# Routing work of VectorE in two parts around the normalisation, and an earlier load of the third expert's weights, in an attention, mixture-of-experts and MLP kernel

## The reference

```python
# attention: 4 batches, 8 heads, 576 positions, head size 64, causal window of 64
scores = (1/8) * q @ k^T, masked to 0 <= i - j < 64
x = softmax(scores) @ v                      # gathered to 2304 tokens x 512
# mixture of experts, 8 experts, 512 -> 1024 -> 512
do_compute = x @ w_skip > 0
e_idx = argmax(x[do_compute] @ w_gate)       # first of equal ones
gate_w = softmax(logits)[e_idx]
y = gate_w * relu(x @ w1[e]) @ w2[e]         # for the tokens of expert e
x = x + y on the tokens with do_compute, x elsewhere
# MLP, 512 -> 2048 -> 512
h = x @ w_in;  out = (h * clip(h + 3, 0, 6) / 6) @ w_out
```

## Time and profile before

| | |
|---|---|
| median of three runs | 718.98 us (718.35 to 719.72) |
| the profiled execution's own time | 716.1 us |
| its span | 714.5 us |
| mean granted TensorE clock | 0.985 |
| TensorE matmul busy | 660.7 us, 92% |
| VectorE busy | 253.6 us, 35% |
| ScalarE busy | 241.3 us, 34% |

### The profile page before, as it was taken

The page is one execution under the profiler, slowest core; times in us unless marked ns, Lnnn a source line. Parts: engine busy times, 40 slices in busy tenths (PEclk is TensorE's granted clock), DMA queues, the critical chain, the costliest instruction groups (busy, mean ns, idle before and its releaser), DMA issues.

```text
span 714.5 us, 17144 instructions
## 1 busy us (share of the span) xinstructions
PE 660.7 (92%) x6662; PEld 580.1 (81%) x6662; DVE 253.6 (35%) x810; ACT 241.3 (34%) x571; POOL 71.6 (10%) x121
## 2 busy tenths in 40 slices
PE   5887776687999999999999999999999999999998
PEld 4776665575788787799989999999999899989996
DVE  2677665400111111265543224322422242224222
ACT  3786766111111111265433223222322232223221
POOL 5224343311111111100000000000000000000000
PEclk9999999898999999999999999999999999999999
DMA  6887768829948335445411002000200020001001
GB/s 151 182 198 176 195 173 281 312 69 380 362 152 304 123 122 201 134 119 147 146 53 38 0 1 89 0 0 0 88 0 0 0 89 0 0 0 44 1 1 44
DMA packets 97251, 78.13 MB, mean 109 GB/s; under 512 B 61793, under 2 KB 76901, under 8 KB 97200
## 3 DMA queue, kind: packets, MB, share of 16 engines
q1 hardware_dynamic: 83392, 43.20, 22.2%
q10 hardware_dynamic: 11360, 30.02, 11.8%
q0 software_dynamic: 2448, 4.22, 1.7%
HBM read 63.23 MB, written 17.52 MB: 113 GB/s over the span
## 4 chain that ended last, share of the span: by engine, by line
PE 79%; DMA 6%; DVE 4%; SPq 4%; issue 3%; ACT 2%; ACTq 1%; POOLq 0%; POOL 0%; DVEq 0%
PE bank L761 28%; PE bank L774 19%; PE av L774 9%; PE av L735 7%; PE bank L724 7%; DMA xin<-x_rows 3%; SPq L364 2%; PE av L621 2%; DMA kraw<-in_k 1%; PE bank L635 1%; ACT pr L820 1%; DVE xall L990 1%; PE bank L569 1%; SPq L372 1%; PE av L694 1%
## 5 line engine op out<-in xcount | busy, mean ns | idle before, releaser
L923 ACT ACTIVATE rel<-bank,half 128x384 f32<-128x384 f32 x96 | 55.7, 580 | 185.2 <-PE bank L761 185.2
L1112 DVE SCALAR_TENSOR_TENSOR act<-rel,bank 128x384 f32<-128x384 f32 x96 | 53.2, 554 | 169.9 <-ACT rel L923 169.9
L761 PE MATMUL bank<-xT_hi,wi_hi 128*128 128x384 f32 x384 | 83.3, 339 | 0.7 <-ACT xT_hi L916 0.7
L761 PE MATMUL bank<-xT_hi,wi_lo 128*128 128x384 f32 x384 | 82.9, 337 | 0.0
L761 PE MATMUL bank<-xT_lo,wi_hi 128*128 128x384 f32 x384 | 82.0, 334 | 0.0
L1116 DVE TENSOR_TENSOR g_lo<-act,g_hi 128x384 fp32r<-128x384 f32 x96 | 53.6, 558 | 67.2 <-ACT g_hi L934 67.2
L774 PE MATMUL bank<-wo_hi,g_lo 128*128 128x512 f32 x192 | 76.2, 397 | 0.0
L774 PE MATMUL bank<-wo_hi,g_hi 128*128 128x512 f32 x192 | 76.1, 396 | 0.0
L774 PE MATMUL bank<-wo_lo,g_hi 128*128 128x512 f32 x192 | 75.8, 395 | 0.0
L761 PEld LDWEIGHTS bank<-xT_hi,wi_hi 128*128 128x128 f32 x384 | 69.0, 188 | 7.7 <-ACT xT_hi L916 0.9
L934 ACT CAST g_hi<-act 128x384 fp32r<-128x384 f32 x96 | 49.3, 513 | 65.5 <-DVE act L1112 65.5
(11 more groups left out here) (123 smaller groups left out, 793.0 us busy)
## 6 DMA issues: line engine op xcount, KB each, us to landing
w1s<-in_moe_w ACTq DMA_DIRECT2D x7, 2048.0 KB, 9.0
w2s<-in_moe_w ACTq DMA_DIRECT2D x7, 2048.0 KB, 15.0
qraw<-in_q SPq DMA_DIRECT2D x36, 128.0 KB, 3.3
kraw<-in_k SPq DMA_DIRECT2D x36, 128.0 KB, 3.7
vnow<-in_v SPq DMA_DIRECT2D x36, 128.0 KB, 3.3
x_new<-xall SPq DMA_DIRECT2D x18, 256.0 KB
out<-ot SPq DMA_DIRECT2D x18, 256.0 KB, 2.1
xn<-x_new SPq DMA_DIRECT2D x17, 256.0 KB, 3.5
```

Of the source, the lines that this page charges most:

```text
L761: last = pe.matmul(bank[f % 4][:, 0:GN], a[:, f, c, :], b[:, c, :], start=(n == 0), stop=(n == 3 * DC - 1))
L923: sc.activation(rel[f % 2][:, :], bank[f % 4][:, 0:GN], ACT.Relu, scale=1.0 / 6.0, bias=half[:, :]).then_inc(s_rel, 1)
L1112: dve.scalar_tensor_tensor(out=act[f % 2][:, :], in0=rel[f % 2][:, :], scalar=1.0, in1=bank[f % 4][:, 0:GN], op0=ALU.min, op1=ALU.mult).th ...
```

## The change

- `choose` is cut in two: `choose` (the maximum, the differences `ldl`, the comparison `leq`) stays before `normalise`; the rest, now `assign` (L1009 to L1014 of before), comes after `normalise` in the same step.
- `place` is cut in two: `count` (for the last group the gate, then the ranks and the running total, L1033 and L1035) stays where `place` was; the rest, still `place` (L1036, L1037, the gate, L1041), comes after `normalise` in the same step.
- The transposed logits of the last three tiles go to banks 2 and 3 instead of bank 7, and no longer wait for `s_x`; `transpose_xs` of the last tile moves behind `logits` in its step.
- At the start, `transpose_qk(1)`, `take_q(1)` and `take_k(1)` move behind the scores, exponentials and score reduction of tile 0.
- ScalarE issues the two weight loads of expert 2 ahead of the loop over the experts, after a wait for `s_xin` to reach 64 (two tiles of `xin` have landed) in place of the wait for `s_scat`; two loads are left after expert 0.

```diff
@@ tensor
             def transpose_lg(T):
                 pe.wait_ge(s_lgs, T + 1)
-                pe.wait_ge(s_x, min(T + 3, NT))
-                if T >= NT - 2:
-                    pe.wait_ge(s_lgc, T)
-                pe.transpose(bank[7][:, LT:LT + P], lgs[:, :], ident[:, :]).then_inc(s_lgt, 1)
+                if T < NT - 3:
+                    pe.wait_ge(s_x, T + 3)
+                else:
+                    pe.wait_ge(s_sm, HP * NT)
+                    pe.wait_ge(s_lgc, T - 1)
+                pe.transpose(lg_bank(T)[:, LT:LT + P], lgs[:, :], ident[:, :]).then_inc(s_lgt, 1)
             transpose_qk(0)
-            transpose_qk(1)
             for T in range(NT + 5):
                 if T < NT:
                     scores(T)
+                if T == 0:
+                    transpose_qk(1)
...
-                if exists(T - 2, NT):
+                if exists(T - 2, NT - 1):
                     transpose_xs(T - 2)
                 if exists(T - 3, NT):
                     logits(T - 3)
+                if T - 2 == NT - 1:
+                    transpose_xs(T - 2)
@@ scalar
             take_q(0)
-            take_q(1)
...
                 if T < NT:
                     exponents(T, 1)
+                if T == 0:
+                    take_q(1)
...
             take_xe()
             sc.wait_ge(s_xst, 16 * NT)
-            sc.wait_ge(s_scat, 16 * NT)
+            sc.wait_ge(s_xin, 64)
+            load_w1(sc, 2, s_wp1[2])
+            load_w2(sc, 2, s_wp2[2])
             for e, first, end in expert_tiles(sc, bounds):
...
                     fixed(sc)
-                    if e == 0:
-                        load_w1(sc, 2, s_wp1[2])
-                        load_w2(sc, 2, s_wp2[2])
                     load_w1(sc, e + 3, s_wp1[e % 3])
                     load_w2(sc, e + 3, s_wp2[e % 3])
@@ vector
                 then(dve.tensor_tensor(leq[:, :, :], logits, top, ALU.is_equal))
+
+            def assign(G):
+                skip = lg[:, :, NE:NE + 1]
                 then(dve.tensor_tensor(lct[:, :, :], leq[:, :, :], tie[:, :, :], ALU.mult))
...
-            def place(G):
-                cols = slice(G * GT, G * GT + GT)
+            def count(G):
                 if G == NG - 1:
                     gate(G)
                 dve.wait_ge(s_rk, G + 1)
...
                 dve.tensor_tensor(cb[:, (G + 1) % 2, :], cb[:, G % 2, :], total, ALU.add).then_inc(s_rkc, 1)
+
+            def place(G):
+                cols = slice(G * GT, G * GT + GT)
                 then(dve.tensor_tensor(rsel[:, :, :], rank[:, :, :], oh[:, 0:GT, :], ALU.mult))
...
             take_k(0)
-            take_k(1)
             for T in range(NT + 5):
                 if T < NT:
                     take_scores(T)
+                if T == 0:
+                    take_k(1)
                 if T % GT == 1 and T >= 2 * GT + 1:
-                    place(T // GT - 2)
+                    count(T // GT - 2)
...
                 if exists(T - 1, NT):
                     normalise(T - 1)
+                if T % GT == 0 and T >= 2 * GT:
+                    assign(T // GT - 2)
+                if T % GT == 1 and T >= 2 * GT + 1:
+                    place(T // GT - 2)
```

More of the change, by code:

```diff
@@ L288, in wait_weights, with lg_bank @@
                 eng.wait_ge(later[e % 3], 16 * ((e - 2) // 3 + 1))
+        def lg_bank(T):
+            return bank[7] if T < NT - 3 else bank[2 + T % 2]
         def w_in_piece(f):
@@ L995, in take_logits @@
                 dve.wait_ge(s_lgt, T + 1)
-                dve.tensor_reduce(lg[:, T % GT, :], bank[7][:, LT:LT + P].rearrange("p (c e) -> p e c", e=LW)[:, 0:NE + 1, :],
+                dve.tensor_reduce(lg[:, T % GT, :], lg_bank(T)[:, LT:LT + P].rearrange("p (c e) -> p e c", e=LW)[:, 0:NE + 1, :],
                                   axis=AX.X, op=ALU.add).then_inc(s_lgc, 1)
```

## The result

The changed kernel takes 699.41 us (median of four runs, 698.91 to 702.35), the kernel before 718.66 in the same measurement (717.31 to 719.72): a ratio of 0.9742, 95% interval 0.971 to 0.9773. The forecast was 700.5 us, within 694 to 709.5.

A forecast was written before the change was run, and what follows sets the result against it. TensorE was taken as the bound, with gains only where it idles or runs at the lower clock. Attention 11.0, its start and end 0.5 and experts 7.0 made 18.5 us, from 718.98 to 700.5 us, range 694 to 709.5.

The forecast's parts named there:

- (a): Attention: the four waits of `values` for VectorE's reduction of the logits go, -12.2 us.
- (b): Attention: `values` and scores after the last stall no longer run at the lower clock, -1.4 us.
- (c): Attention: `choose` no longer holds up the normalisation, so four waits of `transpose_lg` go, -3.1 us.
- (d): Attention: TensorE's `ranks` newly waits for `oh` from the later `assign`, 0.75 us in each of four groups, +3.0 us.
- (e): Attention: `place` behind the normalisation delays the next scores and logits, 0.3 us in each of four groups, +1.2 us.
- (f): Attention: loads of v and k become the next thing late, +1.5 us, between 0 and +6.
- Rival A: Attention: loads become the bound, (f) costs 6 us and not 1.5, time 705.0 us; chance 0.20.
- The experts: Experts: stall and slow second product go, -8.0 us, new `xin` waits +1.0; -7.0 in all, between -2.5 and -8.0.
- Rival B: Experts: early weights hold up `xin` for the fourth tile, TensorE stands 4.5 us, time 705.0 us; chance 0.12.
- Rival C: Experts: `xin` loads pass between the weights' packets, no new wait, 8.0 us instead of 7.0, time 699.5; chance 0.12.
- Rival D: Attention: new waits on `oh` and the logits take the clock down, slower at 729.7 us; chance 0.03.
- Rival E: Attention's stall only passes to `ranks` and the weight queue still holds ScalarE, time 719 us; chance 0.02.

The follow-up runs named there:

- choose_split_only: start_again with `place` whole again, ahead of the logits and the normalisation, so only `choose` is split: 717.92 us, 0.9885 of the kernel before.
- weights_only: The kernel before with only the early issue of the third expert's weights: 718.04 us, 0.9882 of the kernel before.
- place_split_only: start_again with `choose` whole again, ahead of the normalisation, so only `place` is split: 705.65 us, 0.9741 of the kernel before.
- qk_first: start_again with SyncE's queue issuing q and k of tile T + 2 ahead of v of tile T: 702.59 us, 0.9693 of the kernel before.
- again: The changed kernel measured once more without edits, on another chip: 707.03 us, 0.9746 of the kernel before.
- qk_first_new_start: qk_first with the changed kernel's new order at the start of attention: 701.88 us, 0.9686 of the kernel before.
- vector_only: The kernel before with only VectorE's two splits, of `choose` and of `place`: 712.57 us, 0.9819 of the kernel before.
- qk_first_weights_sooner: qk_first with the third expert's weights issued after one tile of `xin` instead of two: 706.64 us, 0.9728 of the kernel before.
- start_again: The changed kernel with the old order at the start of attention, as base for other runs: 705.11 us, 0.972 of the kernel before.

## Why the prediction was right, point by point

The sum was 18.5 us; measured are 19.3 by the medians and 0.0258 of 718.66, 18.5, by the ratio. The sum is right, and so are both large mechanisms. That it agrees so closely is in part luck. In the first profile attention gained less than forecast and the experts more: the four differences of the table make 13.7 us, and the forecast for a profiled execution was 18.5; this execution was the slowest of four. On the other chips, measured one by one, both parts are larger than forecast (13.1 and 8.6 us).

- **(a) the wait for the logits, -12.2.** Right: 1.0 us is left in the first profile, and choose_split_only, which brings it back, loses the whole gain of attention.
- **(b) the clock behind the last stall, -1.4.** Right in kind, too small on the other chips. There attention as before ran at 0.92 and 0.91 of the clock (weights_only, choose_split_only), its twelve steps took 88.1 and 88.2 us instead of 80.8, and the split gained 13.1 us. The step that failed is "after the last of these stalls": the other three stalls can bring the clock down too, and there they did.
- **(c) and (d), -3.1 and +3.0.** Right: idle ahead of `ranks` 0.39, 0.87, 0.88 and 0.99 us in the four groups, 3.1 in all, and place_split_only shows no difference beyond its interval.
- **(e) the next wait for the logits, +1.2.** 1.0 us.
- **(f) the loads, +1.5.** Too small in the first profile. The waits for k in the twelve steps are 2.7 us, and the step with the 1.80 lasted 8.9 us against 5.3 undisturbed: 3.6 in that step alone, half of it clock. With 0.19 and 0.73 of the other two waits that makes 4.5 us. In the profiles of the other chips with this order the waits are 0.6 to 3.3 us. As foreseen, k loads stand on the chain more often: four from 24 to 90 us, landing in 4.05 to 6.55 us, where before there were two, in 4.87 and 4.44. Rival A was the right mechanism at a part of its price; qk_first shows the cause of the waits, the order of the queue.
- **The twelve steps** were to take 69 to 70 us and took 73.3; 3.0 of the missing 3.5 us are (f). On the other chips, with `place` split, they took 70.7 to 74.0, with the unexplained wait of the last section in them, about 2 us.
- **The start, 0.** Not told apart from 0. The +3.93 us of the first profile were its late k load and the clock behind it; in again the mark is reached at 44.59, before at 44.04. Once k comes early the cover is gone and in the one profile of that case the start costs 1.3 to 2.1 us up to step 6 (qk_first_new_start), more than the +0.8 given for it.
- **The end, -0.5.** -0.3 in the first profile. `ranks` waits there for `oh`, 1.79 us at 126.98, as foreseen in kind; the size given was 0.75. On the other chips no gain shows at all: from step 18 to the experts take 24.9 to 26.0 us in the ten profiles with `place` split, and 24.1 and 23.9 in the two with `place` whole. Their clock is lower there (0.73 in again, 0.79 in weights_only). A wait that I can't explain falls just ahead of that stretch (below), so the cause stays open.
- **The experts, -7.0.** Right in mechanism, too small: 9.9 us in the first profile, 8.8 by the profiles of the other chips, 8.6 by the ratio. The stall and the slow product were -7.3 (16.1 us instead of 23.5 for two tiles, with all new waits in it). The working writes 2.9 for the slow product where 6.50 less 3.67 is 2.83; its sum of 8.0 uses the right value. Of the 2.6 us beyond those 7.3, 1.6 are the first product, which ran at the full clock (149.60 to 155.40 before, granted clock 0.71; 145.77 to 150.01 now, 1.00). It goes with neither part of the change: the first product takes 4.25 us in weights_only and in vector_only alike, and 5.80 in place_split_only and qk_first, which have the early weights and the split of `place` together. So it is chance of the execution. A gap of 0.82 us at 186.39 in the fourth tile is gone too, and wasn't traced to an edit. Of both I had said nothing. The wait for `xin`, +1.0, was +0.4.
- **Rival B** would have come true with the weights one tile sooner. The price is 4.2 us, near the 4.5 it was given, at another tile. **Rival C**: the passing is there and the price of nothing is wrong (qk_first_weights_sooner).
- **Rival D** and the last sign of being wrong, a lower clock in attention. In the first profile the sign came true: 0.96 against 1.00 from 25 to 115 us, behind two waits for k. In again and vector_only the clock was 1.00 over this stretch, against 0.92 in weights_only, so there the change raised it. Only in the stretch from step 18 to the experts is it lower with the change, 0.79 against 0.86 in the first pair. **Rival E**, the stall only passed on, did not come: `ranks` waits 3.1 us in the four groups where `values` had waited 12.2.

## What to carry to other kernels

Look for the in-order engine on which a long wait for another engine stands ahead of a short operation that releases the bottleneck, and cut the step so that only what frees the shared buffer stays ahead (here two of the eight instructions of `place`, and the reduction of the logits behind them). Split a stage's work in this way only where a wait stands in it: cutting `choose` moved 3 us from one wait to another. When a stall goes, the next bound is often the order of a DMA queue, where a load that could go stands behind another's wait. And price a stall of TensorE with the clock behind it: where it fell, 3.2 us of waiting cost 4.8 (at 116 us in the trace of before, 0.9 and 0.7 more in the two groups behind it) and 3.59 us cost 6.1 (qk_first_weights_sooner, 2.5 more in one product).

The fastest version found is the changed kernel with q and k issued ahead of v: 0.9685 to 0.9693 of before, where the changed kernel had 0.9742 and 0.9746 and, with the old start, 0.972. The intervals of all of these overlap.

## What was not expected of the hardware

**A wait of VectorE that no engine explains.** In all twelve profiles of the other chips, and in neither of the first measurement, VectorE stands still for some 3.5 us ahead of one normalisation near the end, though `values` had ended about 2 us earlier. In ten of them it is that of the second to last tile, at 112 to 116 us; in weights_only and choose_split_only, the two with `place` whole, it is that of the tile before, at 126 and 128 us. The profile names as releaser only "remote". In again:

```profile
115.34 0.17 DVE L995 TENSOR_SCALAR rse<-av 128x8 f32<-128x8 f32 x1 [3.46 <-remote]
...
116.61 0.30 PE L674 MATMUL av<-ident,lgs 128*128 128x128 f32 x1 [3.34 <-DVE xall L999]
```

The DMA queues of that stretch, 110 to 117 us, hold one packet of each instruction queue beside much traffic (packets, MB, share of the DMA engines' time):

```profile
q1 hardware_dynamic: 1621, 2.08, 83.6%
...
q8 instruction: 1, 0.02, 1.0%
q14 instruction: 1, 0.01, 0.3%
```

That instructions arrived late is a guess; it wasn't tried. The first profile, without the wait, has a packet of q14 in the same stretch and none of q8; around the wait of choose_split_only (122 to 129 us) there is one of q14 and none of q8 as well. So a packet of neither queue goes with the wait.

**The same tile takes longer in the experiments.** From one second product to the next it is 7.7 us in the first profile (166.14 to 173.85) and 8.1 in start_again, though the product itself takes the same 3.67 us:

```profile
146.41 3.67 PE L743 MATMUL av<-w2s,hT 128*64 128x256 f32 x32
154.52 3.67 PE L743 MATMUL av<-w2s,hT 128*64 128x256 f32 x32
```

The experts take 148.8 us in again and 143.6 in the first profile, 5.2 us more, while from the first product of the MLP to the end both take 411.3. The medians of the same kernel are 7.6 us apart (707.03, 699.41); the profiled executions, 703.31 and 702.35, are not typical of either. The difference in a tile is in the first product, at a granted clock of 1.00 both times. Gaps of up to 0.2 us with no releaser appear in some of them, here 0.18 at 152.95, and are half of it at most. Why is open.
